# Splitting the wide TensorE products of a fused attention and two-FFN kernel into two narrower ones

## The reference, cut to what matters

```python
# q, k, v: (4, 8, 576, 64); FFN 1: w_in 512x2048, w_out 2048x512, alpha 2048; FFN 2: the same sizes, no alpha
def reference(q, k, v, moe, moe2):
    attn_out = coarse_attention(q, k, v) + local_attention(q, k, v)   # 144 pooled keys; keys within 3 positions
    x = attn_out.transpose(0, 2, 1, 3).reshape(2304, 512)
    h = x @ w_in
    x = (maximum(h, 0) + alpha * minimum(h, 0)) @ w_out
    h = x @ w2_in
    return where(h > 0, h, exp(minimum(h, 0)) - 1) @ w2_out            # (2304, 512), all in fp32
```

## Time and profile before

| | |
|---|---|
| median of 2 runs | 905.66 us (904.95 to 906.37) |
| profiled execution, its own time | 905.44 us |
| its span, first to last instruction | 903.3 us |
| PE busy | 895.9 us (99%), 6555 matmuls |
| PEld busy | 831.9 us (92%), 6555 loads |
| DVE, ACT, POOL busy | 536.3, 301.3, 281.4 us |
| granted TensorE clock, mean | 1.000 |

### The profile page before, as it was taken

The page is one execution under the profiler, slowest core; times in us unless marked ns, Lnnn a source line. Parts: engine busy times, 40 slices in busy tenths (PEclk is TensorE's granted clock), DMA queues, the critical chain, the costliest instruction groups (busy, mean ns, idle before and its releaser), DMA issues.

```text
span 903.3 us, 17048 instructions
## 1 busy us (share of the span) xinstructions
PE 895.9 (99%) x6555; PEld 831.9 (92%) x6555; DVE 536.3 (59%) x1033; ACT 301.3 (33%) x693; POOL 281.4 (31%) x402
## 2 busy tenths in 40 slices
PE   9999999999999999999999999999999999999998
PEld 7898989999999999999999998888898888889887
DVE  6776567555665354464465576566755657665563
ACT  5643334322422131231322233233432325332233
POOL 5999962222222054463575441100011100000000
PEclk9999999999999999999999999999999999999999
DMA  9985422122210035354272244444454443634411
GB/s 187 202 186 149 127 61 62 48 51 55 69 30 15 16 118 163 105 164 152 82 245 71 74 147 118 118 110 123 148 152 120 117 118 110 194 109 119 121 38 70
DMA packets 117807, 100.80 MB, mean 112 GB/s; under 512 B 63952, under 2 KB 80352, under 8 KB 117728
## 3 DMA queue, kind: packets, MB, share of 16 engines
q1 hardware_dynamic: 116512, 99.41, 39.8%
q10 hardware_dynamic: 1216, 0.30, 0.2%
HBM read 80.29 MB, written 19.40 MB: 110 GB/s over the span
## 4 chain that ended last, share of the span: by engine, by line
PE 73%; DVE 1%; ACT 0%; issue 0%; DVEq 0%
PE ps L269 24%; PE ps L271 24%; PE ps L270 24%; PE ps L581 0%; DVE common L328 0%; PE ps L569 0%; PE ps L557 0%; PE ps L541 0%; PE ps L528 0%; PE ps L549 0%; PE ps L517 0%; DVE xT L737 0%; PE ps L537 0%; ACT xT L1061 0%; DVE stats L719 0%; DVE stats L707 0%
## 5 line engine op out<-in xcount | busy, mean ns | idle before, releaser
L271 PE MATMUL ps<-common,w_hi 128*128 128x384 f32 x768 | 258.2, 336 | 0.0
L270 PE MATMUL ps<-common,w_hi 128*128 128x384 f32 x768 | 258.1, 336 | 0.0
L270 PEld LDWEIGHTS ps<-common,w_hi 128*128 128x128 f32 x768 | 144.6, 188 | 0.0
L271 PEld LDWEIGHTS ps<-common,w_hi 128*128 128x128 f32 x768 | 144.3, 188 | 0.0
L269 PE MATMUL ps<-common,w_out_lo 128*128 128x384 f32 x384 | 133.3, 347 | 0.4 <-DVE common L350 0.4
L269 PE MATMUL ps<-common,w_in_lo 128*128 128x384 f32 x384 | 132.8, 346 | 0.4 <-DVE common L328 0.2
L346 ACT ACTIVATE common<-act_g 128x384 fp32r<-128x384 f32 x96 | 50.5, 526 | 210.5 <-PE ps L271 127.3
L1028 ACT ACTIVATE act_g<-act_g 128x384 f32<-128x384 f32 x96 | 50.5, 526 | 195.1 <-DVE act_g L1024 195.1
L269 PE MATMUL ps<-w_hi,common 128*128 128x512 f32 x288 | 113.6, 394 | 0.0
L271 PE MATMUL ps<-w_hi,common 128*128 128x512 f32 x288 | 113.5, 394 | 0.0
L270 PE MATMUL ps<-w_out_lo,common 128*128 128x512 f32 x288 | 113.5, 394 | 0.0
(11 more groups left out here) (116 smaller groups left out, 1417.4 us busy)
## 6 DMA issues: line engine op xcount, KB each, us to landing
ring<-w_in_parts SPq DMA_DIRECT2D x168, 256.0 KB, 2.6
w_in_parts<-parts SPq DMA_DIRECT2D x8, 1280.0 KB, 5.7
out<-xT SPq DMA_DIRECT2D x18, 256.0 KB, 2.2
xT<-in_moe_w_in SPq DMA_DIRECT2D x16, 256.0 KB, 4.7
xT<-in_moe_w_out SPq DMA_DIRECT2D x16, 256.0 KB, 4.4
raw<-in_moe_w_in SPq DMA_DIRECT2D x16, 256.0 KB, 6.3
w_in_parts<-parts SPq DMA_DIRECT2D x8, 512.0 KB, 3.2
w_stage<-in_moe_w_out SPq DMA_DIRECT2D x16, 256.0 KB, 2.6
```

The costliest lines, as they stand in the source:

```text
L270: pe.matmul(psum, l_hi, r_lo, start=False, stop=False)
L271: return pe.matmul(psum, l_hi, r_hi, start=False, stop=stop)
```

## The change

In the helper, each of the three products is laid as two with half of the moving columns each (192 of 384, or 256 of 512) and the same stationary operand; both write their own half of the bank. Only a product with `start` true stays whole: that is the L269 product of a call that opens a bank. The order is: low by high (one or two pieces), high by low (two pieces), high by high (two pieces). `stop` is set on the very last piece alone, and that piece is returned, so that the semaphore increments hang on it as before. Nothing else is changed: callers, waits, tiles, DMAs and the work of the other engines are the same.

```diff
         def three(pe, psum, left, right, start, stop):
+
             (l_hi, l_lo), (r_hi, r_lo) = left, right
-            pe.matmul(psum, l_lo, r_hi, start=start, stop=False)
-            pe.matmul(psum, l_hi, r_lo, start=False, stop=False)
-            return pe.matmul(psum, l_hi, r_hi, start=False, stop=stop)
+            wide = psum.shape[1]
+            halves = [slice(0, wide // 2), slice(wide // 2, wide)]
+            for cols in [slice(0, wide)] if start else halves:
+                pe.matmul(psum[:, cols], l_lo, r_hi[:, cols], start=start, stop=False)
+            for cols in halves:
+                pe.matmul(psum[:, cols], l_hi, r_lo[:, cols], start=False, stop=False)
+            for cols in halves:
+                last = pe.matmul(psum[:, cols], l_hi, r_hi[:, cols], start=False,
+                                 stop=stop and cols == halves[-1])
+            return last
```

## The result

The changed kernel takes 1,046.63 us (1,046.47 to 1,046.80, 2 runs) for 905.66 us before: 1.156 times as long, 95% interval 1.151 to 1.161. That is 141 us more where 127 were forecast.

A forecast was written before the change was run, and what follows sets the result against it. TensorE's column streaming was taken as the bound, with weight loads hidden beneath it. Terms 91.7 + 32.2 + 3 = 127 us on 905.44 us gave 1,032 us, with a range of 988 to 1,100 for 8 in 10.

The forecast's parts named there:

- What bounds the kernel: TensorE in both FFNs: streaming of the moving columns ends last, 173.0 to 233.4 ns a product, next weight load hidden.
- The counts: Cut products: 2,184 in the first FFN, 840 and 846 in the second; 3,870 more matmuls and loads, some 10,425 of each.
- the steps costed at nothing: Products left whole, instruction issue and fetch, other engines, TensorE's idle time, last copy and store: no time added.
- The half of 192 columns: Both FFNs: pieces spaced by a bare load of 107.5 ns, 215 a pair; adds 91.7 us in the first, 32.2 in the second.
- The two ends around it: Bare float32r load of 128 columns: at 100 ns the kernel takes 984 us, at 120 ns 1,110 us.
- The half of 256 columns: 512-wide products: streams in 116.7 to 120.0 ns, load stays hidden; 0 to 5.6 us more, 3 taken.
- the load isn't what spaces the pieces: Cut products: halves cost only their stream, 0 to 6.6 ns each more; 905 to 931 us, likely near 912; chance 0.06.
- Its other form: Second half of a cut product uses weights already in the array, costing only its stream; 905 to 931 us, shared chance 0.06.
- short streams are cheaper by the column: Cut products: halves stream at bf16's 0.424 ns a column; 47 us less, 858 us; chance 0.02.
- Plain-fp32 pace for narrow products: Cut products: short float32r halves run at 1.94 ns a column, 746 ns a 192-wide pair; 2,635 us; chance 0.04.
- The clock's row: TensorE in both FFNs: row expected unchanged; rival of a lower granted clock doubles streams, about 1,690 us, chance 0.03.
- the rule against it: Skill's N / 2.4 + 2.5 ns formula for cut 384-wide products: 2.5 ns dearer each, an estimate of 8 us for 3,024.

The follow-up runs named there:

- The control with narrow operands: Kernel before with stationary operands of 64 columns instead of 128 in 2,736 products of 384 and 828 of 512, none cut: 903.33 us, ratio 0.998.
- 320 and 64: Kernel before with the 384-column products cut in pieces of 320 and 64 columns, the 512-column ones whole: 1,152.33 us, ratio 1.273.
- the run with thirds: Kernel before with the 384-column products cut in three pieces of 128, the 512-column ones whole: 1,384.37 us, one run.
- the run that repeats the weights less: Changed kernel with all three products done half by half, so the stationary operand follows itself in 2 of 6 places, not 4: 1,046.37 us, ratio 1.156.
- the run with narrow halves: Changed kernel with 64 stationary columns instead of 128 in every cut piece; products with start or stop stay whole at 128: 919.54 us, ratio 1.016.

## Why the prediction was right, and where its sizes were off

**What bounds the kernel** held: TensorE's stream, with the load beneath it. The control with narrow operands shows both halves of it, as shorter loads change nothing and the stream stays.

**The counts** were right to the instruction, and so were the steps costed at nothing. Issue: 12,603 matmuls in the run with thirds still came at the load's pace. The other engines: the second FFN's and the first's extra time is TensorE's own spacing.

**The half of 192 columns** was the deciding step, and its mechanism is shown from four sides: halves and thirds cost the same per piece, 320 and 64 cost more than halves with as many pieces, and with shorter loads the cost of halves goes. The term was mis-sized. It took 107.5 ns for a bare load from three gaps read to 10 ns, and the load in a full queue is 110.8. With the value from the thirds the two terms would have been 2,184 x 48.6 + 840 x 44.9 = 143.9 us and not 123.9. Less the 2.5 us that cutting the 512-wide ones gives back beside cut 384-wide ones (below), that is 141.4; measured were 141.0. The closeness is in part luck. By stages it is 102 us for 106.1 in the first FFN, since beside attention a pair lost less (2 x 113.4 ns for 181.0, where it is 2 x 111.2 for 173.3 without), and 38.5 for 35.2 in the second; the two misses cancel. Nor was the forecast's own miss of 14 us one error: the load's price made it 20 us too low, and the 256-wide halves 5.5 too high. The two ends around it (100 and 120 ns) held. A reader can take from this that a price read from few rounded rows carries 3%, which 6,048 pieces turn into 20 us.

**The half of 256 columns** was costed at 0 to 6.6 ns a pair, with the cause right (the load stays hidden) and the sign wrong: alone it gains 6.7 ns. The step that failed is the assumption that a half streams in no less than half of the whole's time. In the changed kernel less of it arrived: cutting the 512-wide ones as well took 1,049.18 to 1,046.63, 2.5 us, where it took 8 us with whole 384-wide ones around. Two things differ there, and neither is a load of the pieces themselves: the 384-wide products around are cut and can't give their 3.4 us, and a part of the groups does not gain (see the last section).

**The rivals.** That the load isn't what spaces the pieces fell with the thirds, whose 128 columns would have streamed in 57 to 63 ns by the slope and came every 112. Its other form, a second load saved, fell with the load count and the run that repeats the weights less. That short streams are cheaper by the column, the faster rival, was right in a part: the 512-wide products do so, by less than half of the 16 ns supposed there, while the 192-wide ones couldn't show it under their loads. With the loads out of the way they cost 88.8 ns a piece, 2 x 88.8 = 178 for 173 to 177, so they don't gain. Plain-fp32 pace for narrow products is refuted by the same 88.8 ns. The clock's row stayed at the top digit in all slices of all runs.

The Trainium skill, "TensorE: Matmul & The Clock Gate", "Back-to-back issue gap", gives about 81 ns for products of 128 columns with the loads in the stream. For float32r with 128 stationary columns the run with thirds shows 110.8. The formula by which the prediction worked out the rule against it is given there for a single product, and for a stream at 512 columns the section has about 131 ns; the bf16 products at 217 ns agree with the formula and not with that. The same page's section on LDWEIGHTS gives the number of columns divided by 1.2, by which 128 columns take an estimated 107 ns; this case bears that out to 4%.

## What to carry to other kernels

For each product compare two numbers: its stream (its moving columns by the slope read from two widths) and the bare load of its stationary operand, and charge the longer one. Here the two meet at about 250 columns (110.8 / 0.443). The pieces of 64, 128 and 192 columns, all below that, paid a full load each, also where the weights were the same. Read the load's price where a product comes without one ahead of time, and not from the length of its record. Of a product well above that point it is worth measuring whether two halves that both still cover their load are cheaper: here the 512-wide ones were, by 3%, and this one part of the change makes the kernel 0.9% faster.

## What the runs showed that was not expected

Two halves of 256 columns take 226.4 to 226.7 ns where one product of 512 takes 233.4, with two loads for one. It isn't so everywhere. In the changed kernel a group of six such products follows a piece of 192 columns. These are its first two pairs and the product behind it:

```profile
699.71 0.42 PE L273 MATMUL ps<-w_hi,common 128*128 128x256 f32 x2
699.96 0.39 PE L275 MATMUL ps<-w_out_lo,common 128*128 128x256 f32 x2
...
701.09 0.34 PE L273 MATMUL ps<-x_last,ring 128*128 128x384 f32 x1
```

The first pair takes 0.25 us and has the longer record: it carries the wait for the weights whose load began with the piece of 192 before it, some 27 ns. The five behind it take 1.13 us, 226 ns each, so the gain is there, next to cut 384-wide products. A mean over the group (1.38 us for six) hides it. Of the 108 full groups of six in that kernel, 88 have their later pieces spaced by 113 to 115 ns, and 20 by 118, as have all 40 of its full groups of three; at 118 a pair takes 236 ns and nothing is gained.

The run with narrow halves is divided in the same way. Here are two of its groups, and then one of the control, in which nothing is cut; each time the first product of the group and the product behind it:

```profile
700.72 0.39 PE L277 MATMUL ps<-w_hi,common 128*64 128x256 f32 x2
...
702.14 0.34 PE L274 MATMUL ps<-w_hi,ring 128*128 128x384 f32 x1
```

```profile
705.01 0.39 PE L277 MATMUL ps<-w_hi,common 128*64 128x256 f32 x2
...
706.37 0.33 PE L274 MATMUL ps<-w_hi,ring 128*128 128x384 f32 x1
```

```profile
700.85 0.39 PE L277 MATMUL ps<-w_hi,common 128*64 128x512 f32 x1
...
702.25 0.33 PE L274 MATMUL ps<-w_hi,ring 128*128 128x384 f32 x1
```

The first takes 1.42 us for six, 237 ns each, the second 1.36, 227, and whole they take 1.40, 233. Of its 102 full groups 38 are like the second. In the run with only the 512-wide products cut, all 108 have 113 to 115. So the gain comes or fails by the group, in a pattern that repeats from round to round. A cause was not found, and none of the kernels was made to tell.

Whole 384-wide products of the second FFN went from 176.7 to 173.3 ns when only their neighbours were cut to 256; 173 is what such products have in the first FFN, where all are 384 wide. That too is left open.

In a stream bound by loads, a product whose weights are late shows the wait as length of its record: 274 ns for 249 at 192 columns, 391 for 307 at 320, and no idle time.
